# Normalising the attention probabilities before the values, and running the first eight attention units in four sets of banks

## What is computed

```python
for c in range(nc):                       # chunks of 32 tokens
    k_full = [mem_k, k[c_start-16 : c_end+8]]      # 8 + up to 56 keys
    scores = scale * q_c @ k_full.T
    a = exp(scores - max(scores)); a = a / (sum(a) + 1e-9)
    out[c] = a @ v_full
x = out as (3072 tokens, 512)
y = (sigmoid(x @ w_gate) * (x @ w_val)) @ w_out        # 512 -> 1536 -> 512
h = y @ w_in; g = P(h) / (Q(h) + 1e-6)                 # 512 -> 2048, P cubic, Q with |h|
result = g @ w_out2                                    # 2048 -> 512
```

## Time and profile before

| | |
|---|---|
| median of 3 runs | 1199.18 us (1197.22 to 1200.24) |
| the profiled execution: its time, its span | 1198.92 us, 1196.6 us |
| PE busy | 1168.5 us, 98% of the span |
| DVE, ACT busy | 904.0 us (76%), 751.8 us (63%) |
| DMA | 97.79 MB, mean 82 GB/s |
| granted TensorE clock | 0.998 |

### The profile page before, as it was taken

One profiled execution on the slowest core, in us unless ns is written; L12 is line 12 of the kernel. 1 busy time (PEld: TensorE's weight loads), 2 busy tenths in 40 slices (PEclk: granted clock), 3 DMA queues, 4 the chain that ended last, 5 costly groups with the idle time before them and its releaser, 6 DMA issues.

```text
span 1196.6 us, 21070 instructions
## 1 busy us (share of the span) xinstructions
PE 1168.5 (98%) x8160; PEld 957.1 (80%) x8160; DVE 904.0 (76%) x1387; ACT 751.8 (63%) x1224; POOL 120.7 (10%) x150
## 2 busy tenths in 40 slices
PE   8899999899999998999999999999999999999998
PEld 7778888677888866788887888888888888888887
DVE  3686566567666655776558899998998998988987
ACT  2465555455555544555556787877877877877875
POOL 2122322002322200232300000000000000000000
PEclk9999999999999999999999999999999999999999
DMA  8411411742241174332208300200200200200000
GB/s 281 156 53 65 156 54 53 259 144 79 98 168 53 54 256 137 106 132 81 88 18 290 132 1 1 71 1 1 71 0 0 70 0 0 70 0 0 36 1 35
DMA packets 40720, 97.79 MB, mean 82 GB/s; under 512 B 4288, under 2 KB 4288, under 8 KB 40640
## 3 DMA queue, kind: packets, MB, share of 16 engines
q1 hardware_dynamic: 40640, 96.68, 23.6%
HBM read 84.09 MB, written 12.58 MB: 81 GB/s over the span
## 4 chain that ended last, share of the span: by engine, by line
PE 57%; DVE 1%; DMA 1%; SPq 0%; issue 0%; ACT 0%; ACTq 0%
PE ps_h L1263 7%; PE ps_h L1258 7%; PE ps_h L1259 7%; PE ps_y L1302 7%; PE ps_y L1298 7%; PE ps_y L1296 7%; PE ps_h L1152 3%; PE ps_h L1159 3%; PE ps_h L1154 3%; PE ps_y L1197 1%; PE ps_y L1202 1%; PE ps_y L1198 1%; DMA oraw<-wo_l 1%; PE ps_y L1188 0%; PE ps_y L1292 0%; PE ps_y L1290 0%
## 5 line engine op out<-in xcount | busy, mean ns | idle before, releaser
L1152 PE MATMUL ps_h<-xop,wop 128*128 128x512 f32 x504 | 197.2, 391 | 2.9 <-DVE x_raw L809 2.6
L1154 PE MATMUL ps_h<-xop,wop 128*128 128x512 f32 x504 | 196.2, 389 | 0.0
L1159 PE MATMUL ps_h<-xop,wop 128*128 128x512 f32 x504 | 155.9, 390 | 0.0
L1258 PE MATMUL ps_h<-x_split,weights 128*128 128x512 f32 x384 | 149.4, 389 | 0.0
L1259 PE MATMUL ps_h<-x_split,weights 128*128 128x512 f32 x384 | 149.4, 389 | 0.0
L1296 PE MATMUL ps_y<-weights,hid 128*128 128x512 f32 x360 | 140.0, 389 | 0.0
L1298 PE MATMUL ps_y<-weights,hid 128*128 128x512 f32 x360 | 140.0, 389 | 0.0
L788 DVE TENSOR_TENSOR wop<-rawp,wop 128x448 fp32r<-128x448 f32 x144 | 90.9, 660 | 56.6 <-ACT wop L441 56.5
L809 DVE TENSOR_TENSOR x_raw<-ps_h,probs_t 128x512 f32<-128x512 f32 x72 | 49.5, 688 | 87.0 <-PE ps_h L1159 86.6
L675 ACT ACTIVATE tmp<-ps_h 128x512 f32<-128x512 f32 x96 | 57.2, 595 | 92.4 <-PE ps_h L1263 92.4
L1152 PEld LDWEIGHTS ps_h<-xop,wop 128*128 128x128 f32 x504 | 94.6, 188 | 25.3 <-DVE x_raw L809 4.3
(11 more groups left out here) (89 smaller groups left out, 2254.4 us busy)
## 6 DMA issues: line engine op xcount, KB each, us to landing
rawp<-wgv_l SPq DMA_DIRECT2D x36, 512.0 KB, 3.5
oraw<-wo_l SPq DMA_DIRECT2D x72, 256.0 KB, 3.7
unit<-v_l SPq DMA_DIRECT2D x24, 520.0 KB, 5.8
unit<-k_l SPq DMA_DIRECT2D x24, 512.0 KB, 5.7
unit<-q_l SPq DMA_DIRECT2D x24, 256.0 KB, 4.4
x_stage<-y_dram SPq DMA_DIRECT2D x6, 1024.0 KB, 6.0
out<-stage SPq DMA_DIRECT2D x24, 256.0 KB, 2.2
braw<-wb_l SPq DMA_DIRECT2D x11, 512.0 KB, 5.5
```

The source lines that it names most:

```text
L1152: nc.tensor.matmul(dst, w_h[k], xop[:, m, 0, k, :], start=first and k == 0, stop=False, skip_group_check=True)
L1154: nc.tensor.matmul(dst, w_l[k], xop[:, m, 0, k, :], start=False, stop=False, skip_group_check=True)
L1159: last = nc.tensor.matmul(dst, w_h[k], xop[:, m, 1, k, :], start=False, stop=k == 1, skip_group_check=True)
L1258: nc.tensor.matmul(dst, lhs(c, 0), x_split[:, 0, c, :], start=(c == 0), stop=False)
```

## The change

1. **Normalised probabilities.** `normalize(g)` now works on `probs` right after the exponential: the sum over the 64 keys by a reduction, plus 1e-9, reciprocal, product; for the first and last token tile a memset first clears the padded keys. The column of ones goes (v has 64 columns).
2. **Values as weights.** `weigh_values` has 64 keys by 64 values as weights and 32 tokens as moving columns. The result comes out with tokens as columns, in one bank, so the second `turn` goes, and `stage_x` waits for `pv_done`.
3. **The first eight units** use four sets of banks (ps_h and ps_y) and six unit buffers (four of them in the memory of hid1), one unit after another: scores(g), weigh_values(g - 3), turn(g - 2). The warm-up matmuls in and after them go; six products at the very start stay. M1 of the first chain stands before the last weigh_values.
4. **Loads of the start held back.** SP waits for an earlier load to have landed before it issues the next one but one; the second weight load comes after all units.
5. **Middle attentions**: all 36 thirds now lie inside attention (30 before, 6 after it); the work of ACT, DVE and SP between them is put in another order; the load of ACT's sigmoid table moves into the first quad.

```diff
-            wait(dve, xturn_done, g - 1)
+            wait(dve, turned_done, set_before(g))
...
             def normalize(g):
-                b = g % 2
-                ov = ps_att[b][:, :, 0:HP * VD].rearrange("p s (h k) -> p s h k", k=VD)
-                dve.wait_ge(pv_done, g + 1)
-                nc.vector.tensor_scalar(row[b], ov[:, :, :, D], 1e-9, None, ALU.add).then_inc(den_done, 1)
...
+                b, tile = set_of(g), g // B
+                pr = probs[b].rearrange("p h s k -> p s h k")
+                dve.wait_ge(exped, g + 1)
+                if tile == 0:
+                    nc.vector.memset(probs[b][0:CHUNK, :, :, NMEM:NMEM + LEFT], 0.0).then_inc(cut_done, 1)
...
+                nc.vector.tensor_reduce(row[b], pr, AX.X, ALU.add).then_inc(den_done, 1)
...
-                                ps_att[b][CHUNK * c:CHUNK * (c + 1), e, VD * h:VD * (h + 1)],
+                                ps_att[b][D * e:D * (e + 1), 1, P * h + CHUNK * c:P * h + CHUNK * (c + 1)],
+                                v_sb[at][KEYS * e:KEYS * (e + 1), c, h, :],
                                 probs_t[b][KEYS * e:KEYS * (e + 1), h, CHUNK * c:CHUNK * (c + 1)],
-                                v_sb[b][KEYS * e:KEYS * (e + 1), c, h, :], start=True, stop=True)
+                                start=True, stop=True)
...
# SP, start
+            load_qk(0)
+            load_qk(1)
+            load_v(0)
+            qk_here(0)
+            load_qk(2)
+            qk_here(1)
+            load_v(1)
+            v_here(0)
+            load_raw(0)
+            load_qk(3)
+            for g in range(4, UNITS):
+                qk_here(g - 2)
+                load_v(g - 2)
+                v_here(g - 3)
                 load_qk(g)
...
# PE, middle attention
                     scores(a)
+                    if p:
+                        turn(b - 2)
+                    fill()
                     fill()
                     if p:
-                        turn(b - 2, False)
-                    else:
-                        fill()
+                        weigh_values(b - 2)
                     fill()
-                    turn(a, True)
+                    fill()
                     scores(b)
+                    turn(a)
                     fill()
                     fill()
                     weigh_values(a)
-                    turn(b, True)
                     fill()
-                    fill()
-                    weigh_values(b)
-                    turn(a, False)
-                    fill()
+                    if p < UNITS // 2 - 1:
+                        fill()
+                        fill()
+                turn(first + UNITS - 1)
                 fill()
-                turn(first + UNITS - 1, False)
+                fill()
+                weigh_values(first + UNITS - 1)
...
# PE, start
-            warm_up(2 * WARM)
-            attention(0, lambda: warm_up(WARM))
-            warm_up(4 * WARM)
+            warm_up(WARM)
+            for g in range(UNITS):
+                scores(g)
+                if g >= 3:
+                    weigh_values(g - 3)
+                if g >= 2:
+                    turn(g - 2)
+            weigh_values(UNITS - 3)
+            turn(UNITS - 2)
+            weigh_values(UNITS - 2)
+            turn(UNITS - 1)
+            chain(0, -1, range(M1, M2))
+            weigh_values(UNITS - 1)
+            chain(0, -1, range(M2, PROD))
...
# DVE, start, after softmax(g), normalize(g - 1), split_w(0, g - 4) for each unit
+            normalize(UNITS - 1)
+            split_x(0, B11)
+            split_x(0, B21)
+            token_sum(0, T1, 0)
+            token_sum(0, T2, 0)
...
# DVE, middle attention
+                    elif p == 3 and place == 0:
+                        split_wout(n + 9)
+                        split_wout(n + 10)
```

More of the change, by code:

```diff
@@ L319, in _ @@
                 n, g = piece_of(s, 0, TA - 2), UNITS * (s + 1)
+                load_oraw(n + 4)
                 load_qk(g + 2)
-                for ahead in (4, 5, 6):
-                    load_oraw(n + ahead)
+                load_oraw(n + 5)
+                load_oraw(n + 6)
                 load_qk(g + 3)
@@ L336, in _ @@
                 load_oraw(n + 10)
+                load_v(g + 5)
+                load_oraw(n + 11)
                 load_qk(g + 7)
                 load_v(g + 6)
+                load_oraw(n + 12)
                 load_v(g + 7)
-                for ahead in range(11, 16):
+                for ahead in (13, 14, 15):
                     load_oraw(n + ahead)
@@ L915, in last_operands @@
                 between(2)
-            def at_start(p, place):
-                if p == 1:
-                    split_w(0, place)
-                elif p == 2:
-                    split_w(0, 2 + place)
-                    if place:
-                        split_w(1, 0)
-                elif p == 3 and place == 0:
-                    split_x(0, B11)
-                    token_sum(0, T1, 0)
-                    token_sum(0, T2, 0)
-                elif p == 3:
-                    split_x(0, B21)
-                    split_w(1, 1)
-                    split_w(1, 2)
+            for g in range(UNITS):
+                softmax(g)
+                if g:
+                    normalize(g - 1)
+                if g >= 4:
+                    split_w(0, g - 4)
+            normalize(UNITS - 1)
+            split_x(0, B11)
+            split_x(0, B21)
+            token_sum(0, T1, 0)
+            token_sum(0, T2, 0)
             def between(place):
-                if place == 2:
-                    split_w(1, 3)
-            attention(0, at_start)
+                if place < 2:
+                    split_w(1, place)
             last_operands(0, between)
@@ L1120, in warm_up, with chain @@
                     nc.tensor.matmul(ps_y[:, 0, 0:P], ident[:], ident[:], start=True, stop=True)
-            def chain(c, n):
+            def chain(c, n, places=range(PROD)):
                 u, kind = divmod(c, 2)
@@ L1126, in chain @@
                 pe.wait_ge(w_lo, 4 * (c + 1))
-                for m, (w, name, first) in enumerate(STEPS):
+                for m in places:
+                    w, name, first = STEPS[m]
                     if m == M1:
```

266 lines of the change are left out of this document (151 added, 115 removed).

## The result

The change made the kernel slower: 1226.22 us (median of 4 runs, 1224.64 to 1226.75) against 1199.71 for the kernel before (4 runs), ratio 1.0223, 95% interval 1.0205 to 1.0241. The forecast was 1193.5, and 1226 lies above the whole range.

The account below looks back on a forecast made before the run. It took TensorE, busy 98% of the span, as the bound, with gains only where it waits or does other work. Start -13.8, middles +8.0 and clock +0.4 gave -5.4 on 1198.9: 1193.5 us, range 1183 to 1207.

Parts of the forecast that it names:

- W: Time of the new weigh_values on PE, start to next start: 1.0 us, with two places side by side.
- The upper bound, 1.8: weigh_values at 1.8 us if its two places do not overlap; as a rival 1206 us, chance 0.17.
- The middle: Two middle attentions: 32.7 us against 28.7 each, so 4.0 us more, twice.
- DVE sets M4: After the long waits M6 runs at half clock, but VectorE's work times M4; only 0.4 us added in all.
- The three waits: New PE waits in each middle: 4.9 us before M6, 1.6 before the fourth pair's first third, smaller ones 0.6 and 1.0.
- The start, up to normalize(7): First eight units: VectorE and the loads set the pace, and normalize(7) ends at 35.4 us.
- four sets of banks also take up a stall of issue: In the start's units, the extra banks absorb a PE stall like the earlier 2.61 us.
- The rival of the half clock: Without warm-ups PE runs the start at half clock, 4 to 6 us lost, 1198 us; chance 0.15.
- The start, behind normalize(7): VectorE's chain from normalize(7) at 35.4 us to M4 at 57.9, M4 13.8 us earlier than before.
- the term of 2.75 us: Behind the last unit: ScalarE's three high parts, stage_x(7) and split_w(1, 0), for which VectorE waits.
- the last rival: Start not faster than about 5 us, as loads or instruction fetching stall PE every unit; 1202 us, chance 0.08.
- Its tests: Signs of being wrong: weigh_values (L1183) at 1.8 us, clock 0.5 between 8 and 35 us, no middle wait before M6.

Follow-up runs that it names:

- e3: The changed kernel with VectorE's low part that waits for ScalarE moved behind seven sums and low parts of the last operands; 1209.94 us, ratio 1.0074.
- e5: The kernel before with only the change's start (bank sets, buffers, held-back loads), old product form, identity products behind the first three units' scores; 1201.28 us, ratio 0.9998.
- e1: The changed kernel with 6, 6 and 9 identity products behind the first three units' scores; 1225.38 us, ratio 1.0210.
- e2: The changed kernel with each weigh_values product cut in two, 32 values as weights, 128 records; 1239.06 us, ratio 1.0324.
- e6: e3 plus eight identity products ahead of the scores of each of units 1 to 7 of the start; 1205.53 us, ratio 1.0039.
- e14: e6 with three identity products a unit in place of eight; 1207.74 us, ratio 1.0065.
- e12: e5 with e3's edit, the second chain's weights loaded earlier and both chains' weight splits done within the units; ratio 1.0050 to the kernel before.

## Why the prediction was wrong

- **W.** "64 x 28 / 2 = 0.90 ... W = 1.0" failed. It priced a record by its moving columns, from warm-ups in which weights and moving columns are both 128, so the rows could not tell the two apart. Measured: 1.99 at full clock, 3.55 at half. By weights the same row gives it: two cycles a column for 64 columns is 53 ns, two places side by side, 32 x 53 = 1.7, and 1.99 with the gaps. The old form, eight places, lies below its issue pace by either count and could not tell them apart. The upper bound, 1.8, was for the wrong reason and still too low.
- **The middle.** Forecast +4.0, measured +8.2 and +7.2. With W corrected the sum is 32.7 + 8 x 0.99 = 40.6; the waits were 6.8 (4.6, 1.5, 0.7) where it had 11.9 (the first turn, the last turn, M4 and issue cost 0.7 together instead of 5.4), which leaves 35.5. M6 and M5 at half clock took 2.72 and 2.49 us where the kernel before had 1.39 each, 2.4 more, which "DVE sets M4" had put at nothing: M6 to M4 took 10.1 us, 8.2 before. The count is then 37.9 where 28.7 + 8.2 = 36.9 were measured. The three waits were each named with their place, and their sizes held: 4.9 against 4.6, 1.6 against 1.5, 0.6 or 1.0 against 0.7.
- **The start, up to normalize(7).** 35.4 forecast, 53.06 measured. "PE ... 2.5 us a unit, and is covered by DVE's 3.1 to 3.6" failed twice: by W, and by the clock. PE was at half clock for the whole of it, 5.73 us a unit, and "four sets of banks also take up a stall of issue" failed as well: the stop of 3.02 us gave VectorE its longest wait. The rival of the half clock had the mechanism and a chance of 0.15, but a price of 3 us for seven units, since it used W = 2.0 at half clock where 3.55 was measured. Nor was the clock seen to multiply W. The two make most of the 17.7 us: from the scores of unit 3 to those of unit 7, 17.01 to 44.24 us, four units take 27.2 us, 3.7 of them stops of issue, where 3.1 to 3.6 a unit were forecast, 12.4 to 14.4. The against of that rival, "only after a wait of 2.6 us", had a fall of the clock in mind; here it had not risen to begin with.
- **The start, behind normalize(7).** 22.5 us forecast, 29.9 measured. The wait of VectorE for split_w(1, 0) was in the working, but as a chain of 2.75 us behind stage_x(7), with PE's weigh_values(7) taken as covered. PE was last: stage_x(7) waited for it until 65.79. Once PE is late, an order that puts an operation that waits for PE ahead of four that don't makes them late too; e3 shows that this alone was 5.0 us here. In the working's terms, the term of 2.75 us was mis-sized: VectorE's wait there was 7.42.
- **The size of the prize.** Even with the old form (e5), M4 came 2.9 us sooner and not 13.8. That "the fetching of instructions" stalls PE was in the last rival ("start stalled"), which had 0.08; e5's 10.7 us of such stops bear it out for the old form, the 3.02 us of the kernel after for a small part of its loss. No rival had the time behind the last unit.
- **Its tests.** L1183 at 1.8 or more was there at first sight. The half clock between 8 and 35 us was there too, but the page prints 1.00 for it, so this test taken by its words would have passed; only the durations gave it away.

The Trainium skill, "TensorE: Matmul & The Clock Gate", Part 4, says that a transpose does not count as a busy PE in the same way. No run here decides it: in e1, whose clock did not rise, the turns were 1.0 of 5.7 us a unit, and in e5, which has two turns a unit, it rose at 28.2 and 41.8 us.

## What to carry to other kernels

Price a small matmul from both its weights and its moving columns, and take no unit price from rows in which the two are equal: swapping the operands to save a transpose (0.41 us) doubled the weight columns, left two places of eight and cost 1.2 us. Where one engine makes high parts and another low parts, the low part waits for everything ahead of the high one; put behind it whatever needs neither, or, better, in front. Products that only keep the clock up are part of the budget of a start: taking them out is no saving until a profile shows the clock without them. Cutting idle time on PE by dense runs of small products also raises its need of instructions: look at the instruction queue in the DMA view where PE stops without a releaser.

## What the runs showed of the hardware

- A record of 64x64 weights takes 1.99 us / 32 pairs, some 62 ns, with 32 or with 16 moving columns; its weight load stands with 135 ns, that of 32 columns in e2 with 109.
- At half clock a dense stretch of the new form's small products (e1, 9.83 of 10 us busy in its densest part) kept a clock of 0.50 for 40 us; the old form's (e5) saw it rise at 28.2 and 41.8 us; with 16 records of 128x128 in each unit (e6) it was 0.93 to 1.00 from 10 to 60 us; with 6 (e14) PE was at half clock to 20.3 us and had 0.83 to 1.00 after it.
- A printed clock of 1.00 can be wrong ahead of the trace's first record of the clock (64.4 us in the kernel after): there, 64 records of scores took 1.14 us to the next start, as in the 0.50 of e1 (1.11).
- A sum of VectorE that takes 0.68 us took 1.23 beside POOL's sums (e12).
- PE's idle times of issue of 0.85 us and more, 52 in eleven traces, all ended 1.21 to 1.66 us after a 16 KB packet of instructions had landed; the longest was 4.60 us (e2).
